# Wider bonus products, full-height score products and two later waits in a linear attention and mixture-of-experts kernel

## The reference

```
for t in range(S):
    cur = np.einsum('bhd,bhe->bhde', u[None] * kt, vt)
    y[:, :, t] = np.einsum('bhd,bhde->bhe', rt, state + cur)
    state = wt[:, :, :, None] * state + np.einsum('bhd,bhe->bhde', kt, vt)
```

```
logits = x @ w_gate
noisy_logits = logits + np.log1p(np.exp(x @ w_noise)) * noise
for e in range(E):
    for k in range(2):
        h = np.maximum(x[mask] @ w1[e], 0.0)
        out[mask] += top2_w[mask, k, None] * (h @ w2[e])
```

## Time and profile before

| | |
|---|---|
| median of three executions | 1207.7 us |
| profiled execution, its own time | 1206.45 us |
| its span | 1204.9 us |
| mean granted clock of PE | 0.95 |
| end of the last pair's output | 244.47 us |
| PE busy | 1135.9 us (94%) |
| DVE busy | 739.8 us (61%) |

### The profile page before, as it was taken

How to read it: one execution, slowest core, us unless ns; L and a number is a source line. 1 busy time by engine, 2 the same in 40 slices (tenths; PEclk the granted TensorE clock), 3 DMA queues, 4 the chain that set the end, 5 groups by cost and what they waited for, 6 DMA issues and landing times.

```text
span 1204.9 us, 24895 instructions
## 1 busy us (share of the span) xinstructions
PE 1135.9 (94%) x8968; PEld 1082.4 (90%) x8968; DVE 739.8 (61%) x1036; ACT 569.6 (47%) x808; POOL 136.0 (11%) x188
## 2 busy tenths in 40 slices
PE   6899889799889999999999999999999999999998
PEld 5788778789888999999999999889999999999998
DVE  7978888757866767767777667743334343443433
ACT  5434444346436666666666666622332323333232
POOL 1000034141820000000000000220110101101010
PEclk9958787689989999999999999999999999999999
DMA  9744463485777888888888888620110101101010
GB/s 152 121 87 81 81 149 105 155 266 187 246 223 266 277 277 286 273 267 280 279 271 280 278 276 282 206 60 1 59 59 0 59 0 59 55 3 59 0 59 20
DMA packets 192751, 185.04 MB, mean 154 GB/s; under 512 B 98192, under 2 KB 160912, under 8 KB 192688
## 3 DMA queue, kind: packets, MB, share of 16 engines
q1 hardware_dynamic: 176208, 152.74, 44.1%
q0 software_dynamic: 6528, 20.06, 5.0%
q10 hardware_dynamic: 9952, 11.41, 2.7%
HBM read 156.85 MB, written 27.33 MB: 153 GB/s over the span
## 4 chain that ended last, share of the span: by engine, by line
PE 79%; DVE 11%; issue 4%; ACT 3%; SPq 1%; DMA 1%; POOL 1%; ACTq 0%; DVEq 0%; POOLq 0%
PE ps L858 6%; PE ps L859 6%; PE ps L876 6%; PE ps L860 6%; PE ps L877 6%; PE ps L878 6%; PE ps L789 5%; PE ps L791 5%; PE ps L790 5%; PE ps L747 5%; PE ps L749 4%; PE ps L748 4%; PE ps L536 2%; PE ps L551 2%; DVE w_lo L1590 2%
## 5 line engine op out<-in xcount | busy, mean ns | idle before, releaser
L1590 DVE TENSOR_TENSOR w_lo<-w_raw,w_hi 128x1536 fp32r<-128x1536 f32 x140 | 244.6, 1757 | 86.3 <-ACT w_hi L909 86.1
L909 ACT ACTIVATE w_hi<-w_raw 128x1536 fp32r<-128x1536 f32 x140 | 206.6, 1488 | 17.2 <-ACT y_out L1101 12.1
L1590 DVE TENSOR_TENSOR gg<-ps,th 128x768 f32<-128x768 f32 x64 | 61.3, 958 | 168.6 <-ACT th L1148 168.6
L789 PE MATMUL ps<-w_hi,h_hi 128*128 128x384 f32 x440 | 150.0, 341 | 10.7 <-DVE h_lo L1674 8.3
L747 PE MATMUL ps<-xT_hi,w_hi 128*128 128x256 f32 x480 | 140.6, 293 | 10.9 <-DVE xT_lo L1590 5.7
L791 PE MATMUL ps<-w_hi,h_lo 128*128 128x384 f32 x440 | 147.2, 334 | 0.0
L790 PE MATMUL ps<-w_lo,h_hi 128*128 128x384 f32 x440 | 147.1, 334 | 0.0
L1878 POOL DMA_INDIRECT yy<-yg,slot_g x54 | 53.9, 998 | 759.9 <-DVE w_lo L1590 432.8
L748 PE MATMUL ps<-xT_lo,w_hi 128*128 128x256 f32 x480 | 138.0, 287 | 0.0
L749 PE MATMUL ps<-xT_hi,w_lo 128*128 128x256 f32 x480 | 138.0, 287 | 0.0
L876 PE MATMUL ps<-wout_hi,g_hi 128*128 128x384 f32 x384 | 130.4, 340 | 0.0
(11 more groups left out here) (266 smaller groups left out, 2117.7 us busy)
## 6 DMA issues: line engine op xcount, KB each, us to landing
w_raw<-in_moe_w SPq DMA_DIRECT2D x140, 768.0 KB, 4.8
xt_in<-xg SPq DMA_DIRECT2D x20, 384.0 KB, 4.3
yg<-y_out ACTq DMA_DIRECT2D x20, 384.0 KB, 6.0
k_pad<-in_k SPq DMA_DIRECT2D x32, 144.0 KB, 4.0
v_nat<-in_v SPq DMA_DIRECT2D x32, 144.0 KB, 3.6
out<-o_out SPq DMA_DIRECT2D x8, 576.0 KB, 4.0
w_nat<-in_w SPq DMA_DIRECT2D x15, 288.0 KB, 3.5
r_pad<-in_r SPq DMA_DIRECT2D x30, 144.0 KB, 4.0
```

The costliest lines, as they stand in the source:

```text
L789: pe.matmul(o, h_hi[:, f, cols], w2_hi[:, f, :], start=(f == 0), stop=False, skip_group_check=True)
L909: nc.scalar.activation(dst, src, ACT.Copy).then_inc(s, 1)
L1590: vec.tensor_tensor(dst, a, b, ALU.subtract).then_inc(s, 1)
```

## The change

The bonus products write 48 columns for each block instead of two; `usel` has 48 columns for a pair of heads, the last 46 of them zero, and each block's product overwrites what the one before left beyond its own two columns. BAD moves to the last column of the bank. The score products and the products of queries with states run over 64 partitions of a head instead of 48, the padding included. ACT's wait for the cleared rows of `yg` goes from ahead of `two_parts(0)` to ahead of the last pair of tiles. PE makes the table's first row product one step later in whole tile 3, and DVE copies it one step later.

```diff
-        usel = place("usel", [P, HP, 2])
+        usel = place("usel", [P, HP, D])
-        BAD = BETA + 2 * Q
+        BAD = BANK - 1
 def scores(t, p):
-                        rows = slice(HB * h, HB * h + D)
+                        rows = slice(HB * h, HB * (h + 1))
 def betas(p):
-                        mm = pe.matmul(ps[rows, A0, BETA + 2 * q:BETA + 2 * q + 2], kr[:, ...],
+                        mm = pe.matmul(ps[rows, A0, BETA + 2 * q:BETA + 2 * q + D], kr[:, ...],
                                        usel[:, p % HP, :], start=True, stop=True)
 def inter(p):
-                        keys = slice(h * HB, h * HB + D)
+                        keys = slice(h * HB, (h + 1) * HB)
 between, PE:
-                       (3, 0): [lambda: spell(0)], (4, 0): [lambda: spell(1)]}
+                       (3, 1): [lambda: spell(0)], (4, 0): [lambda: spell(1)]}
 ACT:
-            act.wait_ge(y_cleared, 16 * 3)
             tile_act(two_parts(0), one_part(0), 0)
...
+            act.wait_ge(y_cleared, 16 * 3)
             tile_act(two_parts(NSING - 1), one_part(NSING - 1), NST - 1)
 between, DVE:
-                       (3, 1): [lambda: entered(0)], (3, 3): [late[3]], (3, 4): [late[4]], (4, 1): [lambda: entered(1)],
+                       (3, 2): [lambda: entered(0)], (3, 3): [late[3]], (3, 4): [late[4]], (4, 1): [lambda: entered(1)],
```

More of the change, by code:

```diff
@@ L563, in betas @@
                         rows = slice(half * HB, (half + 1) * HB)
-                        mm = pe.matmul(ps[rows, A0, BETA + 2 * q:BETA + 2 * q + 2], kr[:, q * C + half * HB:q * C + (half + 1) * HB],
+                        mm = pe.matmul(ps[rows, A0, BETA + 2 * q:BETA + 2 * q + D], kr[:, q * C + half * HB:q * C + (half + 1) * HB],
                                        usel[:, p % HP, :], start=True, stop=True)
```

## The result

| | before | after |
|---|---|---|
| median of the runs side by side | 1207.76 us (1203.48 to 1208.21) | 1191.07 us (1187.17 to 1193.97, 4 runs) |
| ratio, 95% interval | | 0.9868 [0.9831, 0.9904] |
| profiled execution, its own time | 1206.45 us | 1191.79 us |
| its span | 1204.9 us | 1190.3 us |
| mean granted clock of PE | 0.950 | 0.979 |

A forecast was written before the change was run, and what follows sets the result against it. DVE bounds attention pairs at full clock, PE at half clock. From 1206.45 us, -10.4 - 3.0 - 3.6 - 1.7 + 0.5 = -18.2 us gives 1188.2, stated as 1188.5 us; likeliest case 1185 to 1192, range 1180 to 1201.

The forecast's parts named there:

- clock holds in pairs 3 to 5, -10.4 us: Attention pairs 3 to 5: the clock fall at 59.5 us goes, DVE paces them, 45.00 us becomes 34.6.
- The sign that was to show it: Attention: granted clock full from the start of pair 1 to at least 120 us, pairs 3 to 5 at 11 to 12 us each.
- the case is close: Attention: earlier pairs with the same mix kept the clock, so a little more streamed work should prevent the fall at 59.5 us.
- The later pairs: Attention at 167 to 200 and 214 to 244 us: -3.0 us of 7.2 us of DVE's waits for PE, ends 0 and 7.2.
- The two waits: Whole tile 3's row product and ACT's wait for cleared rows: -3.6 and -1.7 us.
- The row product: Whole tile 3: PE's gap shrinks from 3.30 to 1.1 us with no half clock behind it; -3.6 us, between -1.5 and -4.5.
- The wait for the cleared rows: Ahead of `two_parts(0)`: PE's 1.72 us wait at the down product goes; -1.7 us, between -1.4 and -2.5.
- The columns' price: Bonus products in each attention pair: 3 ns more each at full clock, 5 at half; 0.5 us taken for costs together.
- The fourth rival: Attention: widened products bound by their columns, up to 37 ns more each, clock as it is or lower; 1215 us, chance 0.03.
- The first rival: PE's clock is granted as before because the change does not touch what decides it; -4.8 us, 1201.7 us, chance 0.13.
- The second rival: Attention: the first clock fall only moves to pair 5, 6 or 8, half the gain goes; -11.5 us, 1195 us, chance 0.15.
- The third: Rival: the clock holds more than thought, in later attention pairs too; -23.3 us, 1183 us, chance 0.15.

The follow-up runs named there:

- wide_rows: Kernel before plus 48-column bonus products and 64-partition score and state products, waits not moved: 1201.85 us, ratio 0.9947; repeated on a third chip 1193.33 us, 0.9949.
- before_again: The kernel before, unchanged, run once more on another chip to see how traces differ: 1196.37 us in one execution.
- wide_only: Kernel before with only the bonus products widened to 48 columns: 1201.91 us, ratio 0.9967 [0.9922, 1.0011].
- rows_only: Kernel before with only the score and state products run over 64 rows: 1206.7 us, ratio 0.9979 [0.9958, 1.0000].
- waits_only: Kernel before with only the row product one step later and the cleared-rows wait moved: 1197.69 us, ratio 0.9920; repeated on a third chip 1190.67 us, 0.9934.

## Why the prediction was right, and where it was not

**The direction and the cause of most rows.** In the first pair of traces DVE paces pairs 3 to 5 at full clock where PE did at half; the widened products cost nearly nothing; the waits for PE there go. All of that came as written, to 1 us: pairs 3 to 5 lost 11.4 us against the 10.4 forecast. That the granted clock rises with these edits is shown by the timed runs as well (below).

**The step that failed** is the term "clock holds in pairs 3 to 5, -10.4 us". That the edits raise the clock and so shorten the attention is shown, by `wide_rows` twice, but the term's size and its place were read from one execution, and that execution had the longest fall of six. Over the eleven traces pairs 3 to 5 lost 2.2 us, and 0.3 without the first pair of traces; the rest of the gain lies mostly in pair 0 and in pairs 8 to 15. The sign that was to show it, full clock from pair 1 to 120 us, is in two of the five traces with the edits; the other three have the fall of 3.4 us at some 69 us. The attention edits were forecast at -10.4 - 3.0 + 0.5 = -12.9 us and are worth 6 to 7. The argument "the case is close" fits this and was not carried to its end: the grant came out one way in one execution and another way in the next, and the mean over executions is what is timed. The later pairs, forecast at -3.0, gave -1.9 in pairs 9 to 15. Pair 0 gave -1.8, which was not forecast; the clock is higher there too, by the windows from 13 to 30 us.

**What hid it.** The two waits were forecast at -5.3 us and timed at -7.9, and at -9.7 on the first chip. The row product's steps came as forecast: a gap of 1.13 us, full clock behind it. By the traces it is worth 3.6 to 5.3 us, 4.4 in the mean, near the upper end of its range. The wait for the cleared rows is worth 3.9 us in most executions, where the range ended at 2.5, because the forecast priced the gap and not the fall of the clock behind it; for the row product it had priced both. The same rule, applied to one gap, was left out at the other, since the first trace happened to show no fall there.

So the time came out right by luck, by two errors of opposite sign, one of 6 to 7 us and one of 2.6 to 4.4. On the first pair of traces a third one helped: the attention gained 15.57 us there and tile 0 gave 8 of them back. On the second chip the same change brought 12.0 us (9.2 to 14.7 by the interval), where the forecast had 18.2.

**The columns' price.** Taken from L591 at 3 ns at full clock, it is 34.6 - 33.3 = 1.3 ns. The forecast put this down to the weight loads' setting the pace; the runs show the flat price and not its reason. The fourth rival, 37 ns, is out at 48 columns. At 96 the products take 290 ns from start to end in place of 249 and 6.7 us of PE in all, and the change is worth 2.3 us less than with 48, by medians; the intervals of the two ratios overlap.

**The first rival**, the clock as before, is out: the mean granted clock over the timed runs on the third chip is 0.971 with the attention edits alone and 0.960 for the kernel before, and on the first 0.968 and 0.956. The runs hardly meet: 0.968 to 0.974 over 8 runs against 0.950 to 0.968 over 30 on the third chip, and 0.964 to 0.972 over 10 against 0.949 to 0.962 over 20 on the first. The moved waits alone leave it where it was, at 0.961 and 0.957. The profiled executions say the same, and PE's busy share over the span fell from 94% to 93% while the clock rose from 0.950 to 0.979 in the first pair of traces. The Trainium skill ("TensorE: Matmul & The Clock Gate", section "What's actually happening") ties the clock to how busy PE has been recently. Read as busy time the traces do not agree with it: PE was at half clock while busy for 36.74 of 37.50 us, and the attention edits, which leave the number and the order of PE's instructions alone, raised the granted clock on two chips. How they raise it no run here tells.

**The second rival**, the fall only put off, describes the kernel before better than the one after: in `before_again` the clock fell for less, in the pairs 3 to 5 and again in 6 and 7 (0.95 and 0.87), with no edit at all. **The third**, a clock that holds in the later pairs too, came in part: 0.82 to 0.89 in the windows behind pair 7, not 1.00.

**What stays open.** First, the late copies in whole tile 0. They are in the profile after the change and, smaller or as large, in the traces of the first chip of the experiments: tile 0 took 32.0 us behind the last pair in `wide_rows`, 30.7 in `wide_only` and in `rows_only` and 25.3 in `waits_only`, against 25.0 to 26.6 in all eight traces of the other two chips, with and without the change. PE's product is done by its modelled end and ACT's copy starts microseconds later. In tile 0 all four of these traces with attention edits have it and the one without them on that chip does not. Whole tile 2 points at the chip instead: from tile 1's output to its own it took 21.31 us in the profile after and 21.9 to 22.7 in all four traces of the first chip, `waits_only` with the old attention among them (22.67), against 19.04 to 19.06 in the other nine. Whether the edits, the chip or chance decide was not settled, and whether the product ended late or only its signal came late cannot be told, since the ends of products in a profile are modelled. Second, how the gain is split between the two halves of the attention edits: the timed intervals of `wide_only` and `rows_only` overlap each other and reach no change. Their mean granted clocks, 0.962 and 0.959 against 0.956 for the kernel before and 0.968 for both together, suggest that each has a part.

## What to carry to other kernels

A stretch at half clock in one trace is one draw. Before a term of the sum is taken from it, see whether a second execution of the same kernel has it; where only one trace is there, give such a term a wide range and a value well inside it. At each gap of PE of two or three microseconds price the gap and also the slower products behind it, whether or not the trace at hand shows them. A product so small that its time hardly grows with its columns can be given more of them at almost no cost (here 1.3 ns each from 2 to 48), and that can raise and steady the clock, but only up to where the columns are paid for (12.9 ns each from 48 to 96). A time that comes out as forecast is no proof of the terms: take the terms apart on a second execution.

## What the runs showed of the hardware

The grant of the clock differs between executions of one program with the same data: the old attention ended between 231.79 and 244.47 us in six traces, and this is 12.7 us in a kernel of 1200. The Trainium skill ("TensorE: Matmul & The Clock Gate", section "What's actually happening") calls the slow stretch at a kernel's start "run-variable" and puts it below 1% of a typical span; here falls in the middle of the kernel vary as well, and by slightly more than that. Products with 128 by 64 weights take 33.3 ns each with 2 columns, 34.6 with 48 and 47.5 with 96 at full clock. Widening them and adding a third more rows to others made the granted clock higher (0.971 against 0.960 in the mean of timed runs on one chip, 0.968 against 0.956 on another) and the end of the attention more even from one execution to the next (3.4 us of spread against 12.7). In six traces PE's gap of 2.0 to 2.7 us at the wait for the cleared rows was followed by 3.4 us at half clock; in a seventh, with a gap of 1.72 us, the clock stayed full. And a copy by ACT that waits for one product alone can start over 5 us after that product's modelled end, as in whole tile 0, for a reason that no row of these traces names.
